# Attention cut into tiles of 128 steps and run between the projections of a feed-forward layer

## What is computed

```python
for t in range(S):                                   # per batch entry and head; k_n is k of norm 1
    y[:, :, t] = einsum('bhd,bhde->bhe', q[:, :, t], state)
    v_old = einsum('bhde,bhd->bhe', state, k_n[:, :, t])
    state = state + beta[t] * outer(k_n[:, :, t], v[:, :, t] - v_old)
x = y.transpose(0, 2, 1, 3).reshape(3072, 384)
h = maximum(x @ w_in, 0.0)                           # 384 -> 2048
x = (h * h) @ w_out                                  # 2048 -> 384
h = maximum(maximum(x @ w1, x @ w2), x @ w3)         # 384 -> 768
out = h @ w_out2                                     # 768 -> 384
```

## Time and profile before

| | |
|---|---|
| median of 3 runs | 1076.29 us (1074.19 to 1081.08) |
| span of the profiled execution | 1076.8 us |
| TensorE, of that busy | 978.7 us (91%), 5820 matmuls |
| VectorE, ScalarE, GpSimd busy | 458.0, 294.3, 332.7 us |
| mean granted clock of TensorE | 0.960 of full speed |

### The profile page before, as it was taken

The page is one execution under the profiler, slowest core; times in us unless marked ns, Lnnn a source line. Parts: engine busy times, 40 slices in busy tenths (PEclk is TensorE's granted clock), DMA queues, the critical chain, the costliest instruction groups (busy, mean ns, idle before and its releaser), DMA issues.

```text
span 1076.8 us, 15750 instructions
## 1 busy us (share of the span) xinstructions
PE 978.7 (91%) x5820; PEld 853.4 (79%) x5820; DVE 458.0 (43%) x783; ACT 294.3 (27%) x479; POOL 332.7 (31%) x390
## 2 busy tenths in 40 slices
PE   4219988989989877999999999999999999999998
PEld 4219988989878755888888888888889898888888
DVE  6896433443333488433434334343442323232221
ACT  4523413232101112332323333233312222221211
POOL 5698868587833999000000000000020000000000
PEclk9659989998998999999999999999999999999999
DMA  8949999999977443100101001010011010101000
GB/s 198 245 90 160 219 182 179 198 179 193 192 157 145 130 132 97 64 11 1 58 0 58 0 0 58 0 58 0 9 50 59 1 59 0 58 0 58 15 15 29
DMA packets 185758, 90.41 MB, mean 84 GB/s; under 512 B 148144, under 2 KB 170160, under 8 KB 184752
## 3 DMA queue, kind: packets, MB, share of 16 engines
q1 hardware_dynamic: 174000, 78.76, 33.9%
q10 hardware_dynamic: 11712, 11.01, 3.4%
HBM read 64.59 MB, written 25.17 MB: 83 GB/s over the span
## 4 chain that ended last, share of the span: by engine, by line
PE 73%; DVE 10%; SPq 9%; DMA 5%; issue 2%; ACT 1%; POOL 0%; DVEq 0%; ACTq 0%
PE psum L81 20%; PE psum L83 20%; PE psum L82 20%; DVE sq_lo L935 3%; DVE sq L933 2%; PE psum L640 2%; PE psum L625 2%; PE psum L665 2%; SPq L363 2%; SPq L360 2%; PE psum L602 2%; DVE sol_f L126 2%; PE psum L588 1%; DMA v_t<-in_vn 1%; PE psum L580 1%
## 5 line engine op out<-in xcount | busy, mean ns | idle before, releaser
L933 DVE TENSOR_TENSOR sq<-relu 128x512 f32<-128x512 f32 x96 | 86.7, 903 | 150.1 <-ACT relu L1102 150.1
L81 PE MATMUL psum<-sq_hi,wout_hl 128*128 128x512 f32 x288 | 114.3, 397 | 14.8 <-DVE sq_lo L935 14.8
L83 PE MATMUL psum<-x_hi,wb_hl 128*128 128x512 f32 x324 | 126.1, 389 | 0.0
L82 PE MATMUL psum<-x_lo,wb_hl 128*128 128x512 f32 x324 | 126.1, 389 | 0.0
L81 PE MATMUL psum<-x_hi,wb_hl 128*128 128x512 f32 x324 | 126.0, 389 | 0.0
L935 DVE TENSOR_TENSOR sq_lo<-sq,sq_hi 128x512 fp32r<-128x512 f32 x96 | 86.5, 901 | 67.5 <-ACT sq_hi L1107 67.5
L83 PE MATMUL psum<-sq_hi,wout_hl 128*128 128x512 f32 x288 | 113.4, 394 | 0.0
L82 PE MATMUL psum<-sq_lo,wout_hl 128*128 128x512 f32 x288 | 113.3, 394 | 0.0
L81 PE MATMUL psum<-x_hi,win_hl 128*128 128x512 f32 x288 | 112.4, 390 | 0.4 <-DVE state L892 0.4
L532 POOL TENSOR_TENSOR wo_hl<-raw,units_t 128x1152 fp32r<-128x1152 f32 x2 | 4.2, 2107 | 349.8 <-PE psum L83 349.8
L82 PE MATMUL psum<-x_lo,win_hl 128*128 128x512 f32 x288 | 112.1, 389 | 0.0
(11 more groups left out here) (113 smaller groups left out, 1722.6 us busy)
## 6 DMA issues: line engine op xcount, KB each, us to landing
k_bd<-in_kT SPq DMA_DIRECT2D x24, 192.0 KB, 6.0
q_bd<-in_qT SPq DMA_DIRECT2D x24, 192.0 KB, 6.6
kn_bd<-in_kn SPq DMA_DIRECT2D x24, 192.0 KB, 6.7
v_t<-in_vn SPq DMA_DIRECT2D x12, 384.0 KB, 7.3
xT<-y_t ACTq DMA_DIRECT2D x48, 96.0 KB, 2.9
x_raw<-xT SPq DMA_DIRECT2D x6, 768.0 KB, 5.4
x2T<-x SPq DMA_DIRECT2D x6, 768.0 KB, 4.0
x_raw<-x2T SPq DMA_DIRECT2D x6, 768.0 KB, 4.4
```

The source lines that it names most:

```text
L81: nc.tensor.matmul(out, lhs_hi, rhs_hi, start=first, stop=False)
L82: nc.tensor.matmul(out, lhs_hi, rhs_lo, start=False, stop=False)
L83: return nc.tensor.matmul(out, lhs_lo, rhs_hi, start=False, stop=last)
L933: nc.vector.tensor_tensor(e.sq[f % 2][:], e.relu[f % 2][:], e.relu[f % 2][:], ALU.mult).then_inc(s.sq_ready, 1)
```

## The change

Attention becomes 12 chunks of 64 steps over all 32 heads at once, in 6 tiles of two chunks. The first tile is computed alone. The chunks of tile `i + 1` are then computed between the products of the first layer on tile `i`: a tile is 128 steps of the four batch entries, so 512 tokens. A plan of slots (`Plan`) says behind which `up` (even slots) or `down` (odd slots) each part of the attention stands. The two scalings of `k k^T` for tile `i + 2` (`kk`) stand there too.

The two heads of a pair no longer share a 128-column operand. Each has its own product with 64 stationary columns (48 in the update of the state, 32 in the two products for the block beside), over all 128 rows, half of which are zero; the two products of a pair follow each other and write the two halves of the partitions. A kind of product in a chunk is 16 pairs x 2 heads = 32 products ("phase" below): `kk`, `qk`, `k_s`, `x_block`, `g_block`, `f_d`, `y`, `su`. State and new values of a head lie over each other in one operand (`sw`), so y is one product and not two accumulated ones.

y is no longer stored and loaded: `take_y` copies six of each batch entry's heads from PSUM to the next tile of `x_raw`, the other two go there by six small DMAs (`place_last_heads`); the rows of w_in are loaded in the matching order. There is one `relu`, one `sq` and one PSUM bank for `up` where there were two, two and three. The high part of the weights is taken by ScalarE and the low part by GpSimd, in pieces of 384 or 512 columns an instruction. All loops are written out. The first tile's blocks are inverted on VectorE, the others' on GpSimd, as before.

```diff
-GROUPS = 2
-PAIRS = 8
-STEPS = 4
+GROUPS = 1
+STEPS = 2
+PAIRS = BGS * BP
...
+Plan = namedtuple("Plan", "kk_even kk_odd ks_even fd_even y_even ks_odd fd_odd y_odd sums root norms")
+FIRST_PLAN = Plan(1, 10, 13, 15, 18, 21, 23, 26, 27, 28, 29)
+LATER_PLAN = Plan(1, 4, 7, 9, 12, 15, 17, 20, 23, 26, 29)
...
+            def place_last_heads(i):
+                sp.wait_ge(s.y_ready, 4 * (i + 1))
+                for h in range(2):
+                    for j in range(KD):
+                        sp.dma_start(d.x_raw[64 * h + HD:64 * h + 64, j, :],
...
+            def qk(c, b0):
...
+                for p in range(PAIRS):
+                    for h in range(2):
+                        last = nc.tensor.matmul(square_out(b0, p, 1 - h), d.kz[:, h, p, :], d.qa[:, h, p, :], start=True, stop=True)
...
+            def x_block(c, b):
...
+                        last = nc.tensor.matmul(bank[64 * h + HALF:64 * h + 64, b, p * HALF:(p + 1) * HALF], d.ob[:, p, :], d.f1[:, h, p, :],
...
+            def attention(i, h):
+                a, g = i + 1, i + 2
+                if a > LAST:
+                    return
+                ca, cb, at = 2 * a, 2 * a + 1, plan_of(i)
+                if h == at.kk_even and g <= LAST:
+                    kk(2 * g, 6)
+                if h == at.kk_odd:
+                    if g <= LAST:
+                        kk(2 * g + 1, 6)
+                    x_block(ca, 4)
+                if h == at.ks_even:
+                    k_s(ca)
+                    g_block(ca, 5)
+                    x_block(cb, 4)
+                if h == at.fd_even:
+                    f_d(ca)
+                    qk(ca, 6)
+                if h == at.y_even:
+                    y(ca)
+                    su(ca)
+                if h == at.ks_odd:
+                    k_s(cb)
+                    g_block(cb, 5)
+                if h == at.fd_odd:
+                    f_d(cb)
+                    qk(cb, 6)
+                if h == at.y_odd:
+                    y(cb)
...
+            qk(0, 0)
+            x_block(0, 4)
+            g_block(0, 5)
+            f_d(0)
+            x_block(1, 2)
+            pe.wait_ge(s.sw_zero, 1)
+            y(0)
+            su(0)
+            k_s(1)
+            g_block(1, 3)
+            qk(1, 0)
+            f_d(1)
+            y(1)
+            su(1)
...
+            for n in range(UPS + LAG):
+                if n < UPS:
+                    up(n)
+                    attention(n // KF1, 2 * (n % KF1))
+                if n >= LAG:
+                    down(n - LAG)
+                if n < UPS:
+                    attention(n // KF1, 2 * (n % KF1) + 1)
```

More of the change, by code:

```diff
@@ L81, in three_products @@
     nc.tensor.matmul(out, lhs_hi, rhs_hi, start=first, stop=False)
[L82 to L83 removed]
+    nc.tensor.matmul(out, lhs_lo, rhs_hi, start=False, stop=False)
+    return nc.tensor.matmul(out, lhs_hi, rhs_lo, start=False, stop=last)
 def unit_matrix(eng, ops, link_sem, at, f, zero, one):
@@ new lines, in k_s @@
+            def k_s(c):
+                pe.wait_ge(s.kz_in, 32 * (kz_load(c, True) + 1))
+                pe.wait_ge(s.s_ready, 2 * c)
+                pe.wait_ge(s.y_ready, 2 * c)
+                if c % 2 == 0 and c + 4 <= CHUNKS:
+                    pe.wait_ge(s.cg_ready, min(c + 4, CHUNKS))
+                for p in range(PAIRS):
+                    for h in range(2):
+                        last = nc.tensor.matmul(thin_out(6, p, h), d.kz[:, h, p, :], sw_of(h, p), start=True, stop=True)
+                last.then_inc(s.ks_done, 1)
@@ new lines, in g_block @@
+            def g_block(c, b):
+                pe.wait_ge(s.xt_ready, 2 * (c + 1))
+                pe.wait_ge(s.fz_in, 64 * (c + 1))
+                if c > 1:
+                    pe.wait_ge(s.s_ready, 2 * c)
+                for p in range(PAIRS):
+                    for h in range(2):
+                        last = nc.tensor.matmul(bank[64 * h:64 * h + HALF, b, p * HALF:(p + 1) * HALF], d.xt[:, p, :], d.fz[:, h, p, HALF:CH],
+                                                start=True, stop=True)
+                last.then_inc(s.g_done, 1)
@@ new lines, in f_d @@
+            def f_d(c):
+                pe.wait_ge(s.g_ready, 2 * (c + 1))
+                pe.wait_ge(s.d_ready, c + 1)
+                if c == 1:
+                    pe.wait_ge(s.s_ready, 2)
+                elif c > 1 and c % 2 == 0:
+                    pe.wait_ge(s.xt_ready, 2 * (c + 2))
+                for p in range(PAIRS):
+                    for h in range(2):
+                        last = nc.tensor.matmul(thin_out(4, p, 1 - h), d.fz[:, h, p, :], d.d_t[:, p * HD:(p + 1) * HD], start=True, stop=True)
+                last.then_inc(s.fd_done, 1)
@@ new lines, in y @@
+            def y(c):
+                pe.wait_ge(s.w_ready, 2 * (c + 1))
+                pe.wait_ge(s.a_ready, 2 * (c + 1))
+                if c == 0:
+                    pe.wait_ge(s.cg_ready, 4)
+                elif c == 1:
+                    pe.wait_ge(s.d_ready, 2)
+                for p in range(PAIRS):
+                    for h in range(2):
+                        last = nc.tensor.matmul(y_out(h, p), sw_of(h, p, CH), d.qa[:, h, p, :], start=True, stop=True)
+                last.then_inc(s.y_done, 1)
@@ new lines, in su @@
+            def su(c):
+                pe.wait_ge(s.kn_in, 32 * (c + 1))
+                for p in range(PAIRS):
+                    for h in range(2):
+                        last = nc.tensor.matmul(thin_out(4, p, h, HD), d.nz[:, h, p, :], sw_of(h, p), start=True, stop=True)
+                last.then_inc(s.su_done, 1)
+            def attention(i, h):
+                a, g = i + 1, i + 2
+                if a > LAST:
[25 more added lines that the diff above has]
+                    y(cb)
+                    if a < LAST:
+                        su(cb)
@@ L693, in up @@
+            for c in range(4):
+                kk(c, 2 * c)
+            qk(0, 0)
[12 more added lines that the diff above has]
+            su(1)
+            def up(n):
+                i, f = n // KF1, n % KF1
+                if i == 0 and f % FC == 0:
                     pe.wait_ge(s.wt_ready, 2 * (f // FC) + 1)
-                if not (first and f < NH):
-                    pe.wait_ge(s.relu_ready, KF1 * i + f - NH + 1)
@@ L779, in pass_two @@
                         out_of(t, range(KF2))
-            pass_two(0, True)
-            with pe.Fori(1, TPASS) as i:
+            for i in range(CYCLES):
                 pass_two(i)
@@ L920, in _ @@
-            for g in range(GROUPS):
-                start_cycle(CYCLES - 2 + g, NBLK - 1, g, False)
-                scan(CYCLES - 2 + g, g)
+            take_kk(0, 0)
+            take_kk(1, 2)
+            sums(1, True)
+            norms(1)
+            take_kk(2, 4)
+            take_kk(3, 6)
+            scale_v(0)
+            dve.wait_ge(s.solb_in, 16)
+            substitute(dve, nc.vector, s.dve_link, 2, d.sol_b, d.sol_f, (d.relu[:, 0:256], d.sq[:, 0:256]), one, s.solved)
+            take_qk(0, 0)
```

1415 lines of the change are left out of this document (692 added, 723 removed).

## The result

The changed kernel takes 955.1 us, median of 4 runs (954.54 to 955.97), beside 1078.68 us (1074.19 to 1081.32) for the kernel before on the same chip: a ratio of 0.8851, 95% interval 0.8824 to 0.8878. The profiled execution has a span of 954.0 us. The forecast was 962.

A forecast was written before the change was run, and what follows sets the result against it. TensorE was taken to bound the layers, VectorE the first layer's first pass. Start 115 + first layer's products 391.7 + attention 143.4 + waits 7.5 + VectorE beside GpSimd 6 + second layer 298.8 = 962 us; 8-in-10 range 930 to 1035.

The forecast's parts named there:

- Price of a phase: TensorE, attention: paired halves run side by side; wide phases 1.86 us, thin ones 1.4, the middle of 1.0 and 1.86.
- The changes between forms: TensorE in the first layer: switching to a wider column form costs 0.17 us each, 9.4 us in all.
- Waits: First layer: 1.5 us of waits a tile, 7.5 us for five, plus 6 us for VectorE beside GpSimd.
- The 6 us that I had charged for VectorE beside GpSimd's weight splits: First layer: VectorE and GpSimd slow each other while weight pieces are split; 4 us for some 20 us, charged as 6.
- rival A: First layer held up by waits on VectorE or SP's queue, 30 to 60 us more: 992 to 1022; chance 0.18.
- Start: Before the first `up`: landing at 31, inversion's end at 65 to 68, 115 us in all, between 105 and 123.
- Second layer: Same products in the same order, its edit costed at nothing: 298.8 us.
- B: All phases: products no cheaper than the fastest seen, 3.5 us a phase, 280 instead of 143: 1099 us; chance 0.09.
- D: All phases: weight loads do not overlap, wide 3.5 and thin 1.75 us, 244 us in the layer: 1063; chance 0.03.
- point of decision: Phases in the layer: from a mean of 3.2 us on, the change's sign is decided.
- C's floor: Phases of all kinds cost 2.0 to 2.8 us, 163 to 225 us in the layer: 982 to 1043; chance 0.12.
- E: Start much longer through DMA queues or a cold clock, 15 to 40 us more: 977 to 1002; chance 0.08.

The follow-up runs named there:

- experiment 1: Changed kernel with the two loops of every phase exchanged: all 16 products on the lower half of the partitions, then 16 on the upper; 1067.08 us, ratio 0.9888.
- experiment 4: Changed kernel with the first tile's sums of squares, root and norms moved to earlier slots (20, 22, 25); 952.66 us, ratio 0.8835.
- Experiment 2: Changed kernel with all attention parts of a tile in one slot, nothing of the layer between its phases; 1066.97 us, ratio 0.9915.
- experiment 11: Version 9 with weight pieces 3 to 5 issued behind the last heads and the next chunk's loads, and rounded later; 953.87 us, ratio 0.8852.
- version 7: Version 5 with weight pieces 3 and 4 loaded behind the second chunk's loads, so the store of inverse blocks goes first; 940.72 us, ratio 0.8729.
- experiment 3: Changed kernel with GpSimd's first squares and weight splits moved out of VectorE's first inversion; 952.71 us, ratio 0.8842.
- versions 5: Changed kernel with GpSimd out of the first inversion, first tile's sums earlier, and three of six head transfers on ScalarE's queue; 944.7 us, ratio 0.8769.
- versions 9: Version 7 with weight pieces 3 to 5 issued behind `qk(1)`, ahead of the last heads' transfers; 945.04 us, ratio 0.8783.
- version 12: Versions 10 and 11 together, with 8 unused products ahead of `x_block(0)` and 4 behind `y(1)`; 949.63 us, ratio 0.8812.
- version 10: Version 9 with unused products in the start's waits: 6 ahead of `x_block(0)`, 2 ahead of `y(1)`, 5 behind it; 942.76 us, ratio 0.8759.
- version 8: Version 7 with 27 products of unused result in the start's waits, 16 of them ahead of `x_block(0)`; 947.3 us, ratio 0.8791.

## Why the prediction was right, point by point

**Price of a phase: right, and the mechanism is shown.** The rule read from two rows (a pair on the two halves costs the longer of moved and loaded columns) gave 1.86 for wide phases; the trace has 1.88 to 2.02, 108.1 us for 57 with `su` at 1.44 (106.0 forecast). `su` is cheaper than I said, as both its sides have 48 columns: 48/64 of 1.88 is 1.41. I had overlooked that, and its 3.8 us hid a good part of the error in the other wide phases, which cost 5.9 us more than forecast. The rule also has the answer for the thin ones: I took the middle, 1.4, for caution, where 1.0 was its own value and 1.0 to 1.14 was measured; 21 us against 28. Their 64 passes in 1.04 us are 0.016 us each. The Trainium skill, "TensorE: Matmul & The Clock Gate", Back-to-back issue gap, has an issue floor of about 25 ns for products of up to 64 moving columns; here, with products on two halves, the passes are closer. On one half (experiment 1) they are not: 1.95 us for 64 are 0.030 each.

The changes between forms cost 0.2 us at the first product behind each of 39 slots, 8 us, beside 9.4 forecast for 55 changes. Sum 137 us; with 4 us for the cold clock (4.8 us at the layer's start and 3.5 us at tile 1's ran at 0.50, half the rate) 141. The whole is 536.5 - 391.7 = 144.8 of TensorE's time; forecast 143.4. Some 4 us I can't assign. That the two sums lie 1.4 us apart is luck in part: the thin phases came out 7 us below forecast, and the cold clock and the unassigned rest, 8 us together, were in no term.

**Waits: 7.6 us of idle time in the layer, 13.5 forecast.** 4.4 of them lie in tile 0, 0.69 for a `relu` and 3.71 at its end for the split of x. The 6 us that I had charged for VectorE beside GpSimd's weight splits did not come: no product of tile 0 waited for `sq_lo`. What came instead, the sums and norms ahead of the split of x (experiment 4), was in no term. Tiles 1 and 2 have 0 and 0.3: no slot was missed, and rival A (992 to 1022) did not occur. Experiment 2 shows that the waits exist and are long, 19 us a tile, when nothing covers them. One reading was wrong and cost nothing here: GpSimd's inversion of a tile is 34 us by its busy time, but its operations depend on each other and it lasted 46.9 us (158.19 to 205.06, in tile 0). It was done 3.4 us before tile 1 began, not 20. In experiment 11, where it ended 9.5 us later than in version 7, that margin was gone.

**Start: 111.3, forecast 115.** The inversion ended at 64.3, forecast 65 to 68; the detail was good by luck. The landing came later than the 31 I had placed (32.9). The 10 us that GpSimd's squares and splits cost the inversion (experiment 3) were in my term without my knowing: the 34.2 us that I carried over the earlier trace rows had GpSimd's squares beside them too (its pairs of operations at 38.95, 56.46 and 59.33 took 2.89, 2.94 and 4.64 us, where their neighbours take 0.3 to 0.5). Behind it two errors cancel: `x_block(0)` began 5.6 us after the inversion's end, where I had 9.3 for the store and the load, and the chain from there on took 41.5 us, not 38, for I had left its two `x_block` (1.94 and 1.85 us) out.

**Second layer: 298.6, forecast 298.8.** Tile 5 took 71.0 and not 65.3: two `down` of tile 4 fall into it (4.1), which I had not counted there, and 1.6 are waits and entry.

**Rivals.** B and D (1099, 1063) were the cases in which something does not overlap. Experiment 1 makes B's, halves that do not: 1067 us with mean phases near 3.0, so the point of decision (a mean phase of 3.2 us) was well placed. The rule of the Trainium skill, "TensorE: Matmul & The Clock Gate", Part 3, The mechanism, under which D stood, is borne out neither by the earlier trace rows nor by these phases. Even on one half a pass of experiment 1 takes 3.67 / 64 = 0.057 us, the price of one side, and not of load plus product. C's floor (2.0 to 2.8 for all phases) is refuted by the thin phases. E (start 126 or more) did not occur.

## What to carry to other kernels

Price small products by pairs: if two of them use different halves of the partitions, write them one after the other and count columns, not instructions; in the wrong order the same work costs nearly twice as much. Such phases pay in full only when an engine that is busy anyway has other products to put between them; cheap products alone or good cover alone would each have left this kernel at about 1067 us. And after the chain has been shortened, ask which shorter wait was in the shadow: here moving one load freed a store and stopped instructions, freed those and stopped the head transfers, freed these and delayed the next inversion, and only the first of the three moves was worth keeping.

## What the runs showed of the hardware

- **VectorE goes in step with GpSimd.** Operations with two inputs in SBUF last as long as the GpSimd instruction beside them: 2.80 against 2.75 us, 1.27 against 1.27, each 0.2 us by itself (experiment 3). The earlier trace rows have the like in the kernel before.
- **Short transfers pay for the bytes issued before them**, whatever queue they are on. A store of 512 KB let its reader go after 2.7 us alone and after 8.85 behind two weight pieces (1.5 MB); a placement of six times 32 KB took 2.0 us alone and 8.0 to 8.9 behind three (2.3 MB).
- **TensorE's own instructions are such a transfer.** It stopped after the 26th record of `qk(1)` for 0.63, 1.86 and 4.05 us in the changed kernel and versions 5 and 7. With no weights issued shortly before, there was no stop there in versions 9, 11 and 12, and one of 0.62 in 10. The place goes by the count of instructions and not by the phase: counted from `x_block(0)`'s wait, with the added products, the stop comes behind 538 passes in version 7 (the 26th of `qk(1)`), 538 in version 8 (the 54th of `g_block(1)`, stop of 2.00 us) and 537 in version 10 (the 9th of `qk(1)`). The two other stops of version 8 lie 127 passes ahead of it and 127 behind it, and 127 passes with their weight loads are 254 instructions. In the longest gap the DMA engines' share was 1.08; in that of 1.86 it was 0.07, just behind a stretch of 1.0. The profile's page has a queue for instructions (72 packets, 1.18 MB). The Trainium skill, "Runtime: NRT & Kernel Launch", Instruction fetch mechanics, has the refill in blocks of 16 KiB (256 instructions) by DMA, "mostly hidden"; 1.18 MB in 72 packets and the distance of 254 agree, and here it was not hidden. So the stops belong to the stream of instructions; that the fetch waits behind the weights' bytes is inferred, no run tried it alone, and the gap of 1.86 stays unexplained in its length.
- **The granted clock falls in waits of the start, and products whose result is not used raise it too.** With them `x_block`, `g_block`, `f_d` took 1.21, 1.21, 2.07 us (version 8) instead of 1.92, 1.92, 3.66 (version 7); with 3.79 us of idle time ahead of it (version 10) `x_block` was back at 1.92 and a granted clock of 0.50, with 1.77 (version 12) it took 1.24 at 1.00. The length of the wait alone does not decide: behind 2.1 us of it `k_s` took 2.07 us in version 7, 2.81 in the changed kernel and 3.34 in version 8.
